# A fused attention and two-layer kernel: one copy fewer per token tile, and two operand splits placed ahead of the last softplus groups

## What is computed

```python
def _attn_ref(q, k, v):                     # (4, 8, 576, 64) each
    k_p = k.reshape(B, H, Sp, pool, D).mean(axis=3)
    v_p = v.reshape(B, H, Sp, pool, D).mean(axis=3)
    scores = scale * np.matmul(q, k_p.transpose(0, 1, 3, 2))
    scores = scores - np.max(scores, axis=-1, keepdims=True)
    attn = np.exp(scores)
    attn = attn / (np.sum(attn, axis=-1, keepdims=True) + 1e-09)
    return np.matmul(attn, v_p)

def _moe_ref(x, w_in, w_out):               # x (2304, 512), w_in (512, 2048), w_out (2048, 512)
    h = x @ w_in
    g = np.where(h >= 1, h, np.where(h <= -1, 0.0, (h + 1) ** 2 / 4.0))
    return g @ w_out

def _moe2_ref(x, w_in, w_out):
    h = x @ w_in
    g = np.maximum(h, 0.0) + np.log1p(np.exp(-np.abs(h)))
    return g @ w_out
```

## Time and profile before

| | |
|---|---|
| median of 3 runs | 874.66 us (871.52 to 879.52) |
| the profiled execution | 878.52 us, its span on the core 876.7 us |
| TensorE matmuls | 857.9 us busy (98%), 5182 |
| VectorE | 602.8 us (69%) |
| ScalarE | 491.2 us (56%) |
| GpSimd | 360.7 us (41%) |
| the chain that ended last | 86% TensorE, 7% VectorE |
| the h pairs of layer 1 | 484 to 685 us |
| layer 1's products | 685 us to the end |

### The profile page before, as it was taken

One profiled execution on the slowest core, in us unless ns is written; L12 is line 12 of the kernel. 1 busy time (PEld: TensorE's weight loads), 2 busy tenths in 40 slices (PEclk: granted clock), 3 DMA queues, 4 the chain that ended last, 5 costly groups with the idle time before them and its releaser, 6 DMA issues.

```text
span 876.7 us, 13039 instructions
## 1 busy us (share of the span) xinstructions
PE 857.9 (98%) x5182; PEld 832.6 (95%) x5182; DVE 602.8 (69%) x642; ACT 491.2 (56%) x700; POOL 360.7 (41%) x289
## 2 busy tenths in 40 slices
PE   8889999999999999999999999999999989999998
PEld 7667989999999999999999999999999989999998
DVE  4985666642223478768767599889899999678642
ACT  2575666554444554434535677887888645354532
POOL 6856567665546530000000198898875520000000
PEclk9676999999999999999999999999999999999999
DMA  8850576646555698554551334665655698645532
GB/s 182 212 126 25 145 229 198 197 159 214 198 198 172 202 374 306 190 211 163 202 192 49 96 126 146 228 228 196 228 174 179 206 376 327 234 173 211 192 119 73
DMA packets 106540, 167.83 MB, mean 191 GB/s; under 512 B 21872, under 2 KB 94448, under 8 KB 101872
## 3 DMA queue, kind: packets, MB, share of 16 engines
q1 hardware_dynamic: 93800, 157.86, 53.7%
q10 hardware_dynamic: 12680, 9.14, 3.6%
HBM read 96.21 MB, written 70.78 MB: 190 GB/s over the span
## 4 chain that ended last, share of the span: by engine, by line
PE 86%; DVE 7%; ACT 2%; DMA 2%; POOL 2%; issue 1%; SPq 0%; ACTq 0%; DVEq 0%
PE ps L1255 40%; PE ps L1273 36%; PE ps L1171 2%; PE ps L1207 2%; PE ps L1190 2%; DVE t_a L1049 2%; DMA ops<-gops 2%; DVE ops L1061 1%; PE ps L1288 1%; PE ps L1151 1%; PE ps L1313 1%; DVE den L932 1%; DVE t_a L1052 1%; DVE xs L989 1%; PE ps L1320 0%
## 5 line engine op out<-in xcount | busy, mean ns | idle before, releaser
L1255 PE MATMUL ps<-xs,W 128*128 128x384 f32 x2304 | 408.0, 336 | 0.0
L1255 PEld LDWEIGHTS ps<-xs,W 128*128 128x128 f32 x2304 | 400.2, 188 | 5.2 <-issue 4.6
L1273 PE MATMUL ps<-xs,Tm 128*128 128x384 f32 x1968 | 345.9, 336 | 3.3 <-DVE xs L989 2.8
L1273 PEld LDWEIGHTS ps<-xs,Tm 128*128 128x128 f32 x1968 | 342.2, 189 | 4.2 <-issue 3.4
L731 ACT ACTIVATE xs<-ops 128x768 fp32r<-128x768 f32 (+1 forms) x148 | 111.7, 826 | 158.9 <-PE ps L1273 149.8
L594 POOL TENSOR_TENSOR ops<-ops 128x384 f32<-128x384 f32 x48 | 73.9, 1540 | 305.1 <-DVE ops L1061 221.9
L989 DVE TENSOR_TENSOR xs<-ops,xs 128x768 fp32r<-128x768 f32 (+1 forms) x148 | 130.2, 941 | 1.6 <-ACT xs L731 1.6
L1041 DVE SCALAR_TENSOR_TENSOR ops<-ps,t_a 128x768 f32<-128x768 f32 x48 | 45.9, 956 | 111.8 <-ACT t_a L755 111.6
L753 ACT ACTIVATE t_a<-ps 128x768 f32<-128x768 f32 x48 | 39.0, 813 | 97.2 <-PE ps L1255 97.2
L1074 DVE TENSOR_TENSOR X<-ps,X 128x768 f32<-128x768 f32 x41 | 38.7, 955 | 77.8 <-PE ps L1273 77.8
L1061 DVE TENSOR_TENSOR ops<-t_a,t_b 128x768 f32<-128x768 f32 x48 | 62.8, 1308 | 19.6 <-ACT t_b L774 18.3
(11 more groups left out here) (89 smaller groups left out, 682.5 us busy)
## 6 DMA issues: line engine op xcount, KB each, us to landing
gops<-ops SPq DMA_DIRECT2D x48, 1344.0 KB, 5.8
ops<-gops SPq DMA_DIRECT2D x36, 1536.0 KB, 6.7
X<-gops SPq DMA_DIRECT2D x22, 384.0 KB, 6.4
w_raw<-in_moe_w_in_dram SPq DMA_DIRECT2D x32, 256.0 KB, 3.5
t_raw<-in_moe_w_out_dram SPq DMA_DIRECT2D x6, 1024.0 KB, 10.0
out_dram<-y_out ACTq DMA_DIRECT2D x11, 384.0 KB, 2.9
k_raw<-in_k_dram SPq DMA_DIRECT2D x10, 288.0 KB
q_raw<-in_q_dram SPq DMA_DIRECT2D x20, 144.0 KB, 7.1
```

Of the source, the lines that this page charges most:

```text
L1255: last = mm(banks[:, tb, :], W[:, slot, f, part, c * P:(c + 1) * P], x[:, x_part, at:at + TB], start=c == 0 and s == 0, stop=c == KC - 1 a ...
L1273: last = mm(banks[:, d, :], Tm[:, t, part, j, d * P:(d + 1) * P], g[:, g_part, at * TB:(at + 1) * TB], start=at == 0 and s == 0, stop=at = ...
```

## The change

Four edits. (1) `Y_OPS`: product 0 is copied to one block of X per token tile, not two; product 1 writes the block (0, 0) as banks + (0, 1), where it was banks + (0, 0). In both layers. (2) Step 1's four pieces all follow plus_one(45) on ScalarE and softplus(45) on VectorE. (3) Pieces 0 to 2 of step 2 go ahead of log(47) on ScalarE and, behind add_y of step 0, ahead of softplus(47) on VectorE; piece 3 stays behind. (4) On ScalarE, log(45) goes ahead of exp_abs(46), and log(46) between exp_abs(47) and plus_one(47).

```diff
--- before.py
+++ after.py
@@ -77,7 +77,7 @@
 G_PAIR = ((G11, G21), (G12, G22))
 
 FINAL_OF = {1: (0, 0), 4: (1, 1), 5: (0, 1), 6: (1, 0)}
-Y_OPS = (((0, 0, None), (0, 1, None)), ((0, 0, (0, 0)),), ((0, 1, (0, 1)),), ((1, 0, (0, 1)),),
+Y_OPS = (((0, 1, None),), ((0, 0, (0, 1)),), ((0, 1, (0, 1)),), ((1, 0, (0, 1)),),
          ((1, 1, (1, 0)), (0, 1, (0, 1))), ((0, 1, (0, 1)),), ((1, 0, (1, 0)),))
 Y_LAYER = NT * sum(len(ops) for ops in Y_OPS)
 TURN_0 = 2
@@ -841,16 +841,14 @@
                                 hi_w(0, k + 2)
                         else:
                             if a == HPAIRS - 2:
-                                for piece in range(PIECES // 2):
-                                    fill_hi_piece(fill_of(1, NT + 1), piece)
+                                log(a - 1)
                             exp_abs(a)
-                            if 0 < a < HPAIRS - 1:
+                            if a > 0 and a != HPAIRS - 2:
                                 log(a - 1)
                             plus_one(a)
-                            if a == HPAIRS - 2:
-                                for piece in range(PIECES // 2, PIECES):
+                            if a == HPAIRS - 3:
+                                for piece in range(PIECES):
                                     fill_hi_piece(fill_of(1, NT + 1), piece)
-                                log(a)
                     if layer == 1 and k % JJ < PIECES and k // JJ + 1 < NT:
                         fill_hi_piece(fill_of(layer, k // JJ + 1), k % JJ)
                     if k == QUADS - JJ + 4:
@@ -860,10 +858,12 @@
                     if 0 <= k - FIRST_AT < PIECES:
                         fill_hi_piece(fill_of(layer, NT), k - FIRST_AT)
                 if layer == 1:
+                    for piece in range(PIECES - 1):
+                        fill_hi_piece(fill_of(1, NT + 2), piece)
                     log(HPAIRS - 1)
                 for m in range(1, STEPS + 2):
                     if layer < m < STEPS:
-                        for piece in range(PIECES):
+                        for piece in range(PIECES - 1 if layer == 1 and m == 2 else 0, PIECES):
                             fill_hi_piece(fill_of(layer, NT + m), piece)
                     elif layer == 0 and m == STEPS:
                         for piece in range(PIECES):
@@ -1098,14 +1098,15 @@
                             if a < SHARED and a - 1 in FILL_TURNS:
                                 fill_lo_piece(*FILL_TURNS[a - 1])
                         else:
+                            if a == HPAIRS - 1:
+                                add_y(1, 0)
+                                for piece in range(PIECES - 1):
+                                    fill_lo_piece(fill_of(1, NT + 2), piece)
                             softplus(a)
                             if a == HPAIRS - 3:
-                                for piece in range(PIECES // 2):
+                                for piece in range(PIECES):
                                     fill_lo_piece(fill_of(1, NT + 1), piece)
                             total(a)
-                            if a == HPAIRS - 2:
-                                for piece in range(PIECES // 2, PIECES):
-                                    fill_lo_piece(fill_of(1, NT + 1), piece)
                     if layer == 0 and k + 2 < JJ:
                         lo_w(0, k + 2)
                     if k == QUADS - JJ + 5:
@@ -1116,10 +1117,10 @@
                     if layer == 1 and m == STEPS + 1:
                         for d in range(2):
                             add_half(d)
-                    elif m >= 2:
+                    elif m >= (2 if layer == 0 else 3):
                         add_y(layer, m - 2)
                     if layer < m < STEPS:
-                        for piece in range(PIECES):
+                        for piece in range(PIECES - 1 if layer == 1 and m == 2 else 0, PIECES):
                             fill_lo_piece(fill_of(layer, NT + m), piece)
                     elif layer == 0 and m == STEPS:
                         for piece in range(PIECES):
```

## The result

| | before | changed |
|---|---|---|
| first comparison, 4 runs each | 873.4 us (871.5 to 879.5) | 890.8 us (885.7 to 890.9) |
| all runs of this study | mean 875.5 us (868.5 to 884.3, 126 runs) | mean 886.4 us (880.4 to 893.1, 17 runs) |
| the profiled execution, its span on the core | 878.52 us, 876.7 us | 890.86 us, 888.7 us |
| step 0 starts | 685.13 us | 689.31 us |
| from step 0 to step 5 | 47.2 us | 55.0 us |

The changed kernel is slower: the ratio is 1.0172 with a 95% interval of 1.0109 to 1.0236 in the first comparison, and 1.0116 (1.0060 to 1.0172) and 1.0132 (1.0081 to 1.0183) in two later ones. It is some 8 to 11 us, where I had said 6. The first median, 890.8 us, lies outside my range of 873 to 887; the medians of the two later comparisons, 886.6 and 884.2, lie inside it.

A forecast was written before the change was run, and what follows sets the result against it. TensorE was taken as the bound, losing 4.6 us where layer 1's products begin, the largest possible gain. Step 5 late by 4.9 plus 0.9 for the clock gave 5.8 us, put on the median 874.66: 880.5 us, range 873 to 887.

The forecast's parts named there:

- The copy: Both layers: six VectorE copies of 0.90 us go; layer 0's three are worth nothing, covered by running matmuls.
- Step 1's pieces: On VectorE, four pieces ahead of total(45) end it 1.8 us later; the X load goes out at 699.7, not 697.94.
- The wait for piece 2: In step 2, ScalarE's wait for piece 2's load, 7.1 us from issue, holds softplus(47); total(47) ends 10.4 us later.
- From total(47) to step 3: VectorE's piece 3, t block difference, add and first piece take from 711.5 to 716.5 us; step 3 starts 1.5 later.
- GpSimd's sums: Quad 23's store follows the end of total(47) by 5.4 us and goes out at 716.9 us.
- Step 4's load: Operand load behind quad 23's store takes 9.2 us, the middle of 6.7 and 11.7; step 4 is 5.1 late.
- t_raw: Load of t_raw, issued at 723.1, lands 10.0 us later; VectorE's sum waits for it, step 5 is 4.9 late.
- The clock: Gaps of 2.4, 1.9 and 3.5 us; only slow clock behind the third shows, 0 to 1.85 us, half taken: 0.9.
- The range: Whole run, 873 to 887 us: the light case less 3.5 and the heavy one plus 2, for the spread of runs.
- Heavy: Rival, 884.8 us, chance 0.19: transfers at crowded times, or slow clock behind several gaps that no wait covers.
- Light: Rival, 876.5 us, chance 0.18: the queue is so empty by 717 us that each transfer takes its least.
- The other side: Rival, 870.0 us, chance 0.08: piece 2 is there in time, closing step 2's gap, its slow stretch and step 3's gap.

The follow-up runs named there:

- order_only: The changed kernel's queue order with product 0 copied twice as in the kernel before; ratio to before 1.0089 (1.0048 to 1.0129).
- copy_only: The kernel before with only the new table of results (single copies), queue order unchanged; ratio to before 1.0007 (0.9968 to 1.0046).
- step1_split: The changed kernel with VectorE's step 1 pieces as before, two ahead of total(45), two behind total(46); ratio to before 1.0033 (0.9991 to 1.0074).
- no_load: The changed kernel without the load of step 2's third X piece and ScalarE's wait for it (stale numbers); ratios to before 1.0080 and 1.0043.
- early_load: The changed kernel with the third X piece's load issued ahead of quad 22's store; ratios to before 1.0051 and 1.0038.
- piece2_behind: The changed kernel with only pieces 0 and 1 of step 2 ahead of log(47) and softplus(47); ratio to before 1.0005 (0.9976 to 1.0035).
- after_fourth: The changed kernel, unedited, timed anew against the kernel before; ratio 1.0132 (1.0081 to 1.0183), 56.4 us from step 0 to step 5.
- copy_early_both: The kernel before's order with single copies, third X piece's and step 3's operand loads ahead of quad 22's store; ratios to before 0.9968 and 1.0000.
- later_load: The changed kernel with a 1 MB w_out load issued ahead of the third X piece's load; ratio to before 1.0113 (1.0053 to 1.0173).

## Why the prediction was wrong

The direction and the chain up to step 5 were right. What failed are terms of its sum. On the chain, the wait from the X load's issue to ScalarE was taken as 7.1 us and was 8.1; from total(47) to quad 23's store it was 5.4 and became 6.5; step 4's load 9.2 and 9.6. Together they are 2.5 of the 2.9 us by which step 5 came later than the sum of the waits had it, at 55.0 us in place of 52.1. For the clock behind the gap before step 4 I took 0.9 us; it cost 1.6 in three profiles of four and nothing in the first. So a mean of 9.0 us stands against 5.8 forecast. That is 3 of the 10 us between the forecast, 880.5, and the first median, 890.8. The rest was a draw: its four runs had a mean granted clock of 0.966, where the other 13 of the changed kernel have 0.975 and a mean time of 885.4 us, inside the range. In microseconds from step 0's start (the predicted 52.1 is before's 47.2 plus the 4.9 of the prediction):

| | predicted | changed kernel | before |
|---|---|---|---|
| X load for piece 2 issued | 14.6 | 14.6 | 12.8 |
| ScalarE begins piece 2 | 21.8 | 22.7 | 19.9 |
| step 2 goes on | 23.5 | 24.6 | |
| total(47) ends | 26.4 | 27.4 | 16.0 |
| quad 23's store issued | 31.8 | 34.0 | 21.4 |
| step 3 starts | 31.4 | 34.9 | 29.9 |
| step 4 starts | 43.3 | 46.0 | 38.2 |
| VectorE's sum that waits for t_raw | 48.0 | 50.6 | 41.8 |
| step 5 starts | 52.1 | 55.0 | 47.2 |

- **The copy** was left out of the sum. Nearly right: order_only has most of the loss without the new table. But by itself it isn't nothing: copy_only is 1.9 us over before at equal clock.
- **Step 1's pieces.** total(45) 1.8 us later: right, the X load was issued at 14.6 us as predicted. That this 1.8 us reaches the end unshortened was right too, and more (step1_split).
- **The wait for piece 2** as the deciding step: right, shown by no_load, early_load and piece2_behind. Its size, 7.1 us from issue to ScalarE, failed: it was 8.1, 8.0, 8.9 and 8.0 us in the four profiles of the changed kernel, 7.1 and 7.4 in two of before. I took one row where the earlier trace rows had 8.0 as the greatest. The other kernels fall the same way: 8.3 in order_only and in piece2_behind, where VectorE has all four pieces of step 1 ahead of total(45), 7.3 in copy_only and in step1_split, where it has two. So the longer wait comes with that edit and the later issue; the cause isn't tested.
- **From total(47) to step 3** I had 5.0 us, and it took 724.25 - 716.72 = 7.5. This is the term most mis-sized, but it isn't what made step 5 late: behind step 3 TensorE still waits 2.46 us for step 4's operand, whose load goes out behind quad 23's store, whatever step 3 does. I took VectorE's durations for piece 3 (1.01), and for the t block (2.35) from the earlier trace rows, where GpSimd had finished; behind the changed order GpSimd's four sums of quad 23 run at the same time, and the same rows are 1.84 and 3.98 us. The Trainium skill (SBUF — State Buffer, section Who interferes with whom) has the rule: a VectorE instruction with two SBUF inputs contends with a GpSimd instruction that reads SBUF. This trace agrees, 3.98 us against 2.35. In early_load the two rows are 1.85 and 3.98 as well, and in piece2_behind, the changed order with GpSimd done in time, the t block is back at 2.35; GpSimd's last sum and the t block there:

```profile
698.75 0.99 POOL L602 TENSOR_TENSOR ops<-ops 128x384 f32<-128x384 f32 x1
...
703.46 2.35 DVE L1025 TENSOR_TENSOR Tm<-t_raw,Tm 128x1024 fp32r<-128x1024 f32 x2
```

I had seen the effect (two fill pieces of 1.82 and of 3.45 us stood in my own rows) and used it for pieces 0 and 1, but didn't ask who runs beside the last ones once total(47) moves.
- **GpSimd's sums** suffer from the other side, and this is on the chain: 5.4 us from total(47) to the store were 6.5, another 1.1 us in front of step 4's load. In piece2_behind, where VectorE stands idle beside them, they and the issue take 4.1.
- **Step 4's load** 9.2 predicted, 9.6 measured; **t_raw** 10.0 and 10.4. With the X load and the sums: 1.0 + 1.1 + 0.4 = 2.5 of the 2.7 us by which step 4 was later than predicted. This sum is the account of the miss in the profile.
- **The clock.** Half of 1.85 us taken, for step 4 alone. In the first profile step 4 ran at full speed (8.56), in the three others it took 10.15 or 10.16 us, 1.6 more. TensorE of after_fourth, steps 3 and 4:

```profile
725.04 8.57 PE L1274 MATMUL ps<-xs,Tm 128*128 128x384 f32 x48 [1.95 <-DVE xs L989]
736.01 10.15 PE L1274 MATMUL ps<-xs,Tm 128*128 128x384 f32 x48 [2.41 <-DVE xs L989]
```

The one slow stretch inside step 2 ended within waits in all four, as predicted. The one expected behind the gap before step 3 didn't come: step 3 took 8.57 to 8.59 us in all four.
- **The range.** It added 2 and 3.5 us to the outer cases for the spread of a median. Single runs of the kernel before spread over 868.5 to 884.3 us, mostly with the granted clock, and two medians of the changed kernel, 890.8 and 884.2, are 6.6 apart. The three runs of before that I had were spread over 8 us already, and I should have added that in full on both sides. Even with the measured 9.0 us on the mean of all runs of before, 875.5, the forecast would have been 884.5, and the first median 6 above it.
- **Heavy** (10.1 us, 884.8) came close in size, by luck: it rested on crowded transfers (11.7 and 11.4 us; they took 9.6 and 10.4) or on a slow clock behind several gaps that no wait covers (it was one, in three profiles of four). The time that VectorE and GpSimd cost each other, it didn't have. **Light** did not occur. **The other side** needed the load landed in 2.2 us; it took 8. The prediction also said that this load can't be issued before quad 22 is stored; early_load issues it before, since it reads only quads 20 and 21. With the load issued early enough (early_load) the order still didn't gain, so I was also wrong that "all else in the order is sound", and that 4.6 us were to be had: step 3's operand is next in line. The trace of before had it, the ScalarE row at 713.03 shown under copy_only, which waits 4.40 us for that landing. copy_only shows that step 3 can't start before it, so what is won before step 2 comes back before step 3. Only copy_early_both, which moves that load too, gains: 2.7 us.

## What to carry to other kernels

Before work is moved ahead of other work on an in-order queue, ask of each moved instruction what it waits for: a piece that waits for a transfer holds everything behind it, and here the last softplus, its store and two steps' loads cost 6 to 8 us, while the order with the late piece alone cost 1.5. When a block of work is moved in time, take its durations from rows in which the other engines do what they will do then, not from where it stood. Take one term at a time and ask whether it lies on the chain: the most mis-sized one here did not. And where the clock of an early stage is a draw, judge an edit by the length of its own stage in several profiles, or compare runs at equal granted clock; the first comparison, four runs each, showed 17 us where the place has 9.

## What the runs showed of the hardware that was not expected

- The changed kernel starts step 0 anywhere within 13 us (677.5 to 690.2), with a granted clock of 0.50 to 0.79 from 40 to 80 us, and the kernel before at 678.0 and 685.1, in executions that agree within 0.1 us at the place itself (47.2 and 47.2).
- The length of a gap alone doesn't tell whether a slow stretch follows. Behind gaps of 0.3 to 1.1 us the granted clock never fell. The 2.06 us of before was, both times; the 2.35 to 2.41 us before step 4 of the changed kernel were, three times, the 2.46 of its first profile was not. The 2.71 us before step 3 there was not (8.59 us), while behind 3.28 us in copy_only the next 96 matmuls took 2.8 us more than before's, and behind 3.69 us in piece2_behind the next 120 took 2.4 us more than the 120 ahead of it. In after_fourth the 12 matmuls behind a gap of 3.43 us ran at a granted clock of 1.00, and it fell to 0.50 only behind the next gap, of 2.23 us.
- The landing of the same 384 KB differed with what was issued around it: 4.3 us in early_load, where a 1 MB load had gone out 5.7 us ahead of it and nothing behind it for 7 us; 8.0 with a 1 MB and a 1.5 MB load issued right behind it (the changed kernel); 10.2 right behind the 1 MB load (later_load).
